# Attention and two feed-forward layers on one core: the reciprocals' transfers on another queue, and the score matmuls in another order

## The reference

```python
def _attn_ref(q, k, v, centroids):          # batch 2, 8 heads, 768 positions, 64 features
    q_assign = argmax(q_n . c_n); k_assign = argmax(k_n . c_n)     # nearest of 16 centroids
    mask = q_assign[:, :, :, None] == k_assign[:, :, None, :]
    scores = scale * np.matmul(q, k.transpose(0, 1, 3, 2))
    scores = np.where(mask, scores, -1e9)
    attn = np.exp(scores - max(scores)); attn = attn / (sum(attn) + 1e-9)
    return np.matmul(attn, v)
def _moe_ref(x, w1, w2, w3, w_out):         # 1536 tokens, 512 -> 1024 -> 512
    return (((x @ w1) * (x @ w2)) @ w3) @ w_out
def _moe2_ref(x, w_in, w_out):              # 512 -> 2048 -> 512
    h = x @ w_in
    return (h * np.clip(h + 3.0, 0.0, 6.0) / 6.0) @ w_out
```

## Time and profile before

| | us |
|---|---|
| median of 3 runs | 717.29 |
| lowest, highest | 714.6, 717.4 |
| the profiled execution's own time | 714.6 |
| its span in the profile | 712.8 |
| mean granted clock of TensorE | 0.999 of full speed |
| VectorE busy | 468.5 |
| ScalarE busy | 412.9 |
| GpSimd busy | 446.0 |

### The profile page before, as it was taken

How to read it: one execution, slowest core, us unless ns; L and a number is a source line. 1 busy time by engine, 2 the same in 40 slices (tenths; PEclk the granted TensorE clock), 3 DMA queues, 4 the chain that set the end, 5 groups by cost and what they waited for, 6 DMA issues and landing times.

```text
span 712.8 us, 11831 instructions
## 1 busy us (share of the span) xinstructions
PE 704.4 (99%) x4017; PEld 606.5 (85%) x4017; DVE 468.5 (66%) x706; ACT 412.9 (58%) x856; POOL 446.0 (63%) x455
## 2 busy tenths in 40 slices
PE   8999999999999999999999999999999999999998
PEld 6787767676767767999999999999988889998886
DVE  5227666666767775677986779888865548874221
ACT  6317677766777786354555445477754447775333
POOL 4954453553354465996969969788557768853221
PEclk9999999999999999999999999999999999999999
DMA  8648765867766402111002210012212233221202
GB/s 290 184 114 222 173 110 141 192 116 160 160 134 147 111 13 78 64 63 57 14 17 81 69 60 1 30 60 90 75 46 73 74 103 119 75 75 60 72 32 90
DMA packets 41772, 68.50 MB, mean 96 GB/s; under 512 B 10224, under 2 KB 17904, under 8 KB 41712
## 3 DMA queue, kind: packets, MB, share of 16 engines
q1 hardware_dynamic: 33648, 61.86, 32.1%
q10 hardware_dynamic: 8064, 5.88, 3.4%
HBM read 44.07 MB, written 3.19 MB: 66 GB/s over the span
## 4 chain that ended last, share of the span: by engine, by line
PE 89%; DMA 3%; DVE 2%; issue 2%; ACT 1%; ACTq 1%; SPq 0%; POOL 0%; POOLq 0%; DVEq 0%
PE ps L1315 21%; PE ps L1316 21%; PE ps L1317 21%; PE ps L1427 7%; PE ps L1441 7%; PE ps L1415 5%; PE ps L1417 4%; DMA recip_rows<-recips 2%; DVE neg_max L1114 1%; PE ps L1384 1%; ACT probs L772 1%; DMA wo_raw<-in_wo 1%; ACTq L411 1%; PE ps L1401 1%; PE ps L1346 0%
## 5 line engine op out<-in xcount | busy, mean ns | idle before, releaser
L618 POOL TENSOR_TENSOR b_lo<-stage,b_hi 128x512 fp32r<-128x512 f32 x94 | 111.5, 1187 | 101.4 <-ACT b_hi L855 101.1
L1233 DVE TENSOR_TENSOR g_lo<-gate,g_hi 128x384 fp32r<-128x384 f32 x96 | 83.4, 875 | 64.8 <-ACT g_hi L926 64.8
L1114 DVE TENSOR_REDUCE neg_max<-ps 128x1 f32<-128x768 f32 x96 | 89.9, 948 | 36.8 <-PE ps L1417 36.8
L926 ACT CAST g_hi<-gate 128x384 fp32r<-128x384 f32 x96 | 49.2, 514 | 89.8 <-PE ps L1317 89.8
L772 ACT ACTIVATE probs<-ps,neg_max 128x768 f32<-128x768 f32 x96 | 86.8, 906 | 17.6 <-DVE neg_max L1114 17.5
L1427 PE MATMUL ps<-ident,probs 128*128 128x128 f32 x576 | 79.2, 274 | 0.0
L1427 PEld LDWEIGHTS ps<-ident,probs 128*128 128x128 f32 x576 | 67.0, 140 | 11.9 <-issue 6.0
L1135 DVE TENSOR_TENSOR sum_lo<-sum_raw,sum_hi 128x768 fp32r<-128x768 f32 x64 | 65.1, 1020 | 15.4 <-ACT sum_hi L831 15.2
L866 ACT COPY probs_t<-ps 128x512 f32<-128x512 f32 x96 | 54.5, 586 | 35.6 <-PE ps L1427 19.2
L1317 PE MATMUL ps<-b_hi,g_lo 128*128 128x512 f32 x192 | 74.8, 389 | 0.0
L1316 PE MATMUL ps<-b_lo,g_hi 128*128 128x512 f32 x192 | 74.8, 389 | 0.0
(11 more groups left out here) (129 smaller groups left out, 1862.8 us busy)
## 6 DMA issues: line engine op xcount, KB each, us to landing
stage<-in_wio SPq DMA_DIRECT2D x64, 256.0 KB, 2.6
qk_ops<-qk_split SPq DMA_DIRECT2D x32, 384.0 KB, 5.3
stage<-in_w SPq DMA_DIRECT2D x46, 256.0 KB, 3.3
qk_raw<-in_qk SPq DMA_DIRECT2D x16, 384.0 KB, 7.1
qk_ops<-qk_split SPq DMA_DIRECT2D x32, 192.0 KB, 5.0
v_raw<-in_v SPq DMA_DIRECT2D x16, 192.0 KB, 2.7
recip_all<-recip_rows ACTq DMA_DIRECT2D x30, 96.0 KB, 3.2
out<-out_sb ACTq DMA_DIRECT2D x11, 256.0 KB, 2.4
```

Of the source, the lines that this page charges most:

```text
L618: nc.gpsimd.tensor_tensor(b_lo[n % 2][:, cols], stage[n % 2][:, cols], b_hi[n % 2][:, cols].bitcast(F32), ALU.subtract).then_inc(s_lo[half ...
L1114: nc.vector.tensor_reduce(neg_max[:, g:g + 1], scores[g % 2], AX.XY, ALU.max, negate=True).then_inc(s_max, 1)
L1233: nc.vector.tensor_tensor(g_lo[i][:], hidden(q, c, f)[0][:], g_hi[i][:].bitcast(F32), ALU.subtract).then_inc(s_glo, 1)
```

## The change

Stores and spreads of all units are issued by SP. In the loop over heads the store of unit n - 3 stands between `load_ops(n)` and `load_raw(n + 2)`, its spread between `load_mask(n)` and `load_v`. Those of units 13, 14 and 15 follow the loop. ScalarE's queue issues none. In `score`, the four matmuls go half by half: 128 rows and 80 rows of the first half, then of the second; before, both halves' 128-row matmuls came first and then both 80-row ones.

```diff
-        def store_recips(eng, u):
-            eng.wait_ge(s_recip, u + 1)
-            eng.dma_start(recip_rows[u % 2].rearrange("(k p t) -> p k t", k=2, t=3),
-                          recips[:, u * ST:(u + 1) * ST].rearrange("p (k t) -> p k t", k=2)).then_inc(s_rrow, 16)
-        def spread_recips(eng, u):
-            eng.wait_ge(s_rrow, 16 * (u + 1))
-            rows = recip_rows[u % 2]
-            for k in range(2):
-                eng.dma_start(recip_all[k * D:(k + 1) * D, x_cols(u)], rows[k * HALF:(k + 1) * HALF].partition_broadcast(D)
-                              ).then_inc(s_rall[u % 2], 16)
...
         (in the program of SP; the two functions are the same there, with sp for eng)
             for n in range(2, HEADS):
                 load_ops(n)
+                if n >= 3:
+                    store_recips(n - 3)
                 if n + 2 < HEADS:
                     load_raw(n + 2)
                 load_mask(n)
+                if n >= 3:
+                    spread_recips(n - 3)
                 if n % 2 == 1 and n >= 5:
                     load_v(n - 1)
                     load_v(n)
-            store_recips(sp, UNITS - 1)
-            spread_recips(sp, UNITS - 1)
+            for u in range(UNITS - 3, UNITS):
+                store_recips(u)
+                spread_recips(u)
...
         (in the program of ScalarE)
                 if s + 1 < SLOTS:
                     exp(s + 1)
-                if s % ST == 3 and s >= ST:
-                    spread_recips(act, s // ST - 1)
                 if s >= 1 and not groups_first:
                     group_copies(s - 1)
-                if s % ST == 1 and s >= ST:
-                    store_recips(act, s // ST - 1)
...
         (in score, in the program of TensorE)
-                halves_of = [(scores[s % 2][:, half, :], slice(half * HALF, (half + 1) * HALF)) for half in range(2)]
-                for tile, cols in halves_of:
+                for half in range(2):
+                    tile, cols = scores[s % 2][:, half, :], slice(half * HALF, (half + 1) * HALF)
                     nc.tensor.matmul(tile, ops[:, 0, q], ops[:, 2, cols], start=True, stop=False)
-                for tile, cols in halves_of:
                     mm = nc.tensor.matmul(tile, ops[0:MASK_ROWS, 1, q], ops[0:MASK_ROWS, 3, cols], start=False, stop=True)
                 mm.then_inc(s_scores, 1)
```

More of the change, by code:

```diff
@@ L511, in _, with store_recips, spread_recips @@
             load(GATE0 + 1, w12[1])
+            def store_recips(u):
+                sp.wait_ge(s_recip, u + 1)
+                sp.dma_start(recip_rows[u % 2].rearrange("(k p t) -> p k t", k=2, t=3),
+                             recips[:, u * ST:(u + 1) * ST].rearrange("p (k t) -> p k t", k=2)).then_inc(s_rrow, 16)
+            def spread_recips(u):
+                sp.wait_ge(s_rrow, 16 * (u + 1))
+                rows = recip_rows[u % 2]
+                for k in range(2):
+                    sp.dma_start(recip_all[k * D:(k + 1) * D, x_cols(u)], rows[k * HALF:(k + 1) * HALF].partition_broadcast(D)
+                                 ).then_inc(s_rall[u % 2], 16)
             for n in range(2, HEADS):
                 load_ops(n)
+                if n >= 3:
+                    store_recips(n - 3)
                 if n + 2 < HEADS:
```

## The result

| | us |
|---|---|
| after, median (lowest, highest) of 12 runs | 721.66 (719.7, 725.4) |
| before, median (lowest, highest) of 12 runs beside them | 714.42 (713.1, 717.4) |
| ratio after / before, 95% interval | 1.0099 [1.0079, 1.0118] |
| after, the profiled execution's own time, and its span | 723.6, 721.8 |
| after, mean granted clock of TensorE | 1.000 of full speed |

The forecast was no change (716.4, on the scale of a median of 717.29). The kernel loses 7.2 us, twice the 3.6 us that the prediction took as the least a measurement can tell from nothing, and the profiled executions differ by 9.0 us.

A forecast was written before the change was run, and what follows sets the result against it. TensorE's own stream was taken as the bound; 714.6 us - 1.3 (ScalarE's queue) + 0 (late spreads) + 0.4 (score order) = 713.7, or 716.4 on the median's scale; range 712 to 724.

The forecast's parts named there:

- What bounds the kernel: TensorE's stream bounds the attention; the chain's 3% for reciprocals' transfer and ScalarE's queue is mostly not lost time.
- Part 1: ScalarE's queue loses 15 stores and 30 spreads; saves at most 1.3 us of TensorE's waits for the first exp.
- Part 2: SP's queue takes the stores, each costing an issue of 0.56 us at most, hidden before the masks' release: no loss.
- Part 3: Spreads move behind SP's masks; VectorE waits 0.4 to 0.9 us in 13 units, counted as 0, at most 19.5 us.
- the prediction's own sign of being wrong: At SP's spreads: the prediction is wrong if their landing exceeds 3.6 us.
- Its second reason for taking 0: At the spreads: today's long landings come with two queues issuing at once, which the change ends (issue up to 2.53 us).
- there are 1.3 us before TensorE feels anything: Cover for VectorE's late multiply, from the end of the exp behind it to the score matmul's weight load: 1.3 us.
- The rule of the Trainium skill: An SDMA engine alternates between queues, each in order, so spreads behind masks on SP's queue would land later; no size given.
- Part 4: New order of the four score matmuls costs 4 ns a slot, 0.4 us; bounds 9.6 us loss, 0.3 us gain.
- The spreads land late: Rival: spread landings on SP over 3.6 us make TensorE pay in 13 units, 726.2 us on the median's scale; chance 0.18.
- the other three rivals: Alternating score weights costs, 725.6 us (0.08); ScalarE was worth more, 709.0 (0.06); it does nothing, 717.3 (0.06).

The follow-up runs named there:

- e11: Kernel before, with the spreads issued in slot 4 instead of 3 on ScalarE's queue: 714.00 us, ratio 0.9995.
- e12: Kernel before, with spreads in slot 4 of ScalarE's queue, GpSimd's scale_q first, and VectorE's best_rank and reciprocals ahead of the multiply: 714.43 us, ratio 0.9992.
- e6: Kernel before, with only the spreads moved to SP's queue behind the masks, stores staying on ScalarE's queue: 722.67 us, ratio 1.0090.
- e2: Kernel before, with only the order of the four score matmuls changed: 715.07 us, ratio 1.0006.
- e9: Changed kernel with the old score order, and VectorE's best_rank and reciprocals moved ahead of the multiply: 716.21 us, ratio 1.0023 to the kernel before.
- e8: Changed kernel with the old score order, and SP issuing the spreads ahead of the masks: 735.23 us, ratio 1.0269 to the kernel before.

## Why the prediction was wrong, step by step

- **What bounds the kernel: right.** TensorE's stream, with the 3% of the chain for transfer and queue worth little; e11 and e12 took the stand away and gained nothing measurable.
- **Part 1: right.** Saved 1.3 us at most by the forecast; the scores behind P times V came 1.4 us earlier in all, and the probs_t idle time went.
- **Part 2: a size wrong, without effect on the sum.** The store's issue was priced at 0.56 us "at most", though that is the median of the spreads in the earlier trace rows, whose longest issue is 2.53; after, the store's takes 1.71 in the median. First the kernel after, then the kernel before: issues of the store line, in ns (min/median/max).

```profile
L500 SPq DMA_DIRECT2D recip_rows<-recips x16: 365/1714/1809, 71.6 to 284.0; - x16
```

```profile
L403 ACTq DMA_DIRECT2D recip_rows<-recips x15: 361/366/403, 69.1 to 264.5; - x15
```

  The gap of 4.6 us behind it holds that. e6, without the long issue, loses the same within the intervals.
- **Part 3: this is the step that failed, in its cover.** The wait itself was foretold: 13 places, 0.4 to 0.9 us each, against 13 with a mean of 1.25 (0.43 to 2.12). It came out larger in part because the second spread started 4.85 us behind the first mask (mean of 13), not 4.5: in some units the masks' or the first spread's issue took longer. Issues and landings:

```profile
L507 SPq DMA_DIRECT2D recip_all<-recip_rows x32: 444/594/1882, 79.3 to 288.3; - x32
...
DMA to landing us min/median/max: 2.6/2.9/4.0
```

  The 13 second spreads that matter landed in 3.2 us on average (2.7 to 4.0), as the earlier trace rows had it; four of them took over 3.6, the prediction's own sign of being wrong. Its second reason for taking 0, that long issues would end with the two queues' issuing at once, failed as well: with SP alone an issue still takes up to 1.88 us. With a cover of 1.3 us, waits of this size would have cost 2.8 us in all (the excess over 1.3, in seven units), within the forecast's own range. But "there are 1.3 us before TensorE feels anything" was false. I had followed the multiply to its two nearest consumers, the row maxima and P times V. The third goes through another engine's queue (best_rank, mask columns, x_low, scale_q, logits) and has only 0.7 us. Over the eleven units with logits, the waits' excess over 0.66 us sums to 6.3 us, and the idle time seen there is of that size: 4.3 us at the logits and 2.1 at P times V. So the term that was put at nothing measures 8.3 us of TensorE's time (4.5 at the logits, 2.6 at P times V, 1.2 at two transposes).
- **The rule of the Trainium skill** (its page "DMA: Bandwidth & Descriptors", section "Queues, rings and completion order") did not decide it. Spreads behind the masks on SP's queue landed in 2.9 us in the median, against 3.2 on ScalarE's own queue; the second spreads of units 0 to 12 alone took 3.2 us in the mean, against 3.8 before. So this case's trace does not show the longer landing that the prediction drew from the rule. (The rival that it calls the second there is the first of its list.) What made the spread late is the place in SP's program, ahead of the landing.
- **Part 4: right in size.** Against 0.4 us, the trace of e2 has some 0.6 at the score matmuls and their neighbours, and its time differs by 0.4 us, inside its interval; in the trace after it is 1.2.
- **The rivals.** "The spreads land late" had the mechanism and the sign, with 0.18; it set the breaking point at a landing of 3.6 us, whereas by the true slack it lies near 3.0, below what the earlier trace rows showed as the median. With the GpSimd path in view it would have been the forecast. No run shows that the store is part of it (e6), and the other three rivals did not happen.

## What to carry to other kernels

When a transfer is moved, list everything that stands in program order behind the instruction that waits for it, and follow each through the queues of the other engines to the bound engine; the cover is the smallest of the slacks, not that of the nearest consumer. Where a wait can't be made shorter, put the work that doesn't need the data ahead of it (e9: three steps moved, four fifths of the loss back). And before freeing an engine from a stand, ask what the bound engine would do with the time: here one slot later on the same queue (e11) freed it as well, at no cost and for no gain.

## What the hardware showed that was not expected

In e8 a stand of TensorE of 2.8 us was followed by some 6 us of work at half clock (from 177.4 to 183.5), so it cost about twice its length. Of e8's five longest stands, four (2.2, 2.4, 2.8 and 3.1 us) had the granted clock at 0.50 behind or already during them, and one of 2.3 us did not; e11's profiled execution has it too, at a stand of 2.35 us. The changed kernel's stands, under 1 us, left the clock at 1.000.

The issue of the same 3 KB store takes 0.37 us on ScalarE's queue and 1.71 us in the median on SP's directly behind four operand transfers of 192 to 384 KB; the shortest one on SP took 0.365 us. Either of the two spreads behind six mask transfers can take long to issue, the first up to 1.85 us and the second up to 1.88. So a DMA's issue is no constant of the instruction. Standing behind others on the same queue is not the only case: in the kernel before, a spread on ScalarE's queue took 2.53 us at 200.93, while SP issued masks from 200.73 on. What holds an issue up stays open. By contrast, changing the order of 128-row and 80-row weights in the score matmuls made the three distances of starts within a slot longer by 5 to 7 ns together, the middle one going from 175 to 177 or 178, and moved the time by nothing that could be measured.
